# A first wave of 29 steps, and another order of a few loads and copies, in a spectral layer fused with a feed-forward layer

## The reference, cut to what matters

```
X = rfft(x, axis=1)
Yr = Xr @ w_r - Xi @ w_i + b_r ;  Yi = Xr @ w_i + Xi @ w_r + b_i
Y  = soft_threshold(Yr, 0.01) + 1j * soft_threshold(Yi, 0.01)
y  = irfft(Y, n=3008)
h  = y @ w_in
P  = a0 + a1*h + a2*h^2 + a3*h^3 ;  Q = 1 + |b0|*|h| + |b1|*h^2
out = (P / (Q + 1e-6)) @ w_out
```

## Time and profile before

| what | value |
|---|---|
| median of three runs | 1515.61 us |
| profiled execution: its time, its span | 1517.63 us, 1515.8 us |
| TensorE busy (matmuls) | 1452.0 us, 96% |
| VectorE busy | 1272.8 us, 84% |
| ScalarE busy | 1215.2 us, 80% |
| GpSimd busy | 636.8 us, 42% |
| moved by DMA | 187.90 MB, mean 124 GB/s |

### The profile page before, as it was taken

How to read it: one execution, slowest core, us unless ns; L and a number is a source line. 1 busy time by engine, 2 the same in 40 slices (tenths; PEclk the granted TensorE clock), 3 DMA queues, 4 the chain that set the end, 5 groups by cost and what they waited for, 6 DMA issues and landing times.

```text
span 1515.8 us, 19944 instructions
## 1 busy us (share of the span) xinstructions
PE 1452.0 (96%) x6976; PEld 1234.3 (81%) x6976; DVE 1272.8 (84%) x1301; ACT 1215.2 (80%) x1577; POOL 636.8 (42%) x420
## 2 busy tenths in 40 slices
PE   7996999999999999999999999999999999999986
PEld 2885888888888888888888888888888778787775
DVE  0243798888988888889899889989999999999997
ACT  3464788887888787888888888888888888888886
POOL 0000344444444444444444444444455555555554
PEclk9998999999999999999999999999999999999999
DMA  8875465665555655555554564555455544555443
GB/s 249 249 234 134 107 149 119 141 137 128 119 128 123 137 133 112 130 121 103 120 125 94 116 129 102 113 112 125 82 124 102 114 93 92 112 102 107 93 78 68
DMA packets 97682, 187.90 MB, mean 124 GB/s; under 512 B 11120, under 2 KB 57520, under 8 KB 97584
## 3 DMA queue, kind: packets, MB, share of 16 engines
q0 software_dynamic: 29952, 98.58, 35.4%
q1 hardware_dynamic: 67632, 88.05, 20.2%
HBM read 50.54 MB, written 37.49 MB: 58 GB/s over the span
## 4 chain that ended last, share of the span: by engine, by line
PE 65%; DVE 22%; issue 5%; DMA 4%; ACT 1%; SPq 1%; POOL 0%; POOLq 0%; ACTq 0%
PE h_ps L386 21%; PE o_ps L399 7%; PE o_ps L411 7%; PE o_ps L401 7%; DVE num L674 5%; DVE g_hi L666 5%; DVE den L669 5%; DVE num L649 5%; PE d L358 4%; PE d L359 4%; PE d L365 3%; PE d L371 3%; DMA zp_in<-spec 2%; PE d L345 2%; PE d L351 2%
## 5 line engine op out<-in xcount | busy, mean ns | idle before, releaser
L693 POOL TENSOR_TENSOR g_lo<-num,sq 128x940 fp32r<-128x940 f32 (+1 forms) x208 | 453.8, 2182 | 260.7 <-DVE num L674 260.4
L684 POOL DMA_DIRECT2D den<-sq x208 | 182.9, 879 | 612.5 <-PE o_ps L411 318.8
L399 PE MATMUL o_ps<-g_hi,wout_hi 128*128 128x470 f32 (+1 forms) x832 | 330.2, 398 | 0.0
L386 PE MATMUL h_ps<-yt_hi,win_hi 128*128 128x470 f32 (+1 forms) x832 | 312.1, 375 | 3.2 <-DVE num L654 3.2
L386 PE MATMUL h_ps<-yt_lo,win_hi 128*128 128x470 f32 (+1 forms) x832 | 311.5, 374 | 0.0
L386 PE MATMUL h_ps<-yt_hi,win_lo 128*128 128x470 f32 (+1 forms) x832 | 309.4, 372 | 0.0
L401 PE MATMUL o_ps<-g_hi,wout_lo 128*128 128x470 f32 (+1 forms) x832 | 309.1, 372 | 0.0
L411 PE MATMUL o_ps<-g_lo,wout_hi 128*128 128x470 f32 (+1 forms) x832 | 227.6, 395 | 30.1 <-POOL g_lo L693 30.0
L536 ACT ACTIVATE sq<-h_ps,bsq 128x940 f32<-128x940 f32 (+1 forms) x208 | 214.7, 1032 | 50.4 <-POOL g_lo L693 50.2
L666 DVE SCALAR_TENSOR_TENSOR g_hi<-num,a_sb,sq 128x940 fp32r<-128x940 f32 (+1 forms) x208 | 247.3, 1189 | 8.8 <-ACT sq L589 8.2
L674 DVE SCALAR_TENSOR_TENSOR num<-num,a_sb,den 128x940 f32<-128x940 f32 (+1 forms) x208 | 245.7, 1181 | 5.0
(11 more groups left out here) (64 smaller groups left out, 1498.7 us busy)
## 6 DMA issues: line engine op xcount, KB each, us to landing
den<-sq POOLq DMA_DIRECT2D x200, 470.0 KB, 4.4
spec<-s1w SPq DMA_DIRECT2D x64, 192.0 KB, 3.2
z_in<-spec SPq DMA_DIRECT2D x96, 128.0 KB, 3.3
spec<-s_out SPq DMA_DIRECT2D x96, 128.0 KB, 3.3
xw<-in_x SPq DMA_DIRECT2D x31, 384.0 KB, 4.4
out_t<-o_sb SPq DMA_DIRECT2D x25, 470.0 KB, 5.4
zp_in<-spec SPq DMA_DIRECT2D x22, 480.0 KB, 4.9
inv_in<-in_inv SPq DMA_DIRECT2D x96, 64.0 KB, 2.3
```

The source lines that it names most:

```text
L386: mm = pe.matmul(h_ps[q % 2][:, j, 0:cols(q)], w[:, h, f * P:(f + 1) * P], y[t % 2][:, h, 0:cols(q)], start=i == 0, stop=i == len(terms) - 1)
L399: pe.matmul(o_ps[:, h, 0:w], wout_hi[:, f, h * P:(h + 1) * P], g_hi[q % 2][:, j, 0:w], start=f == 0, stop=False)
L693: pool.tensor_tensor(g_lo[r % 2][:, :, 0:cols(r)], ring(num, r), ring(sq, r), ALU.mult).then_inc(n_g, 1)
```

## The change

PRE goes from 28 to 29: the wave has 29 spectral steps, and the slots have 67 (slot 38, the last of tile 4's four, is left empty). Three lists change beside it. SyncE loads w_r, w_i and the bias ahead of the first four z tiles instead of behind them. Of the four x chunks after the wave it issues one at once and three in slot 2, which puts them behind the z load of slot 1. On ScalarE group(1) is ahead of the loop beside group(0), and the copy of S2 of slot 0 is in slot 0, ahead of the reciprocal of slot 0, not at the head of slot 1.

```
-PRE = 28
+PRE = 29
...
-S2_SLOTS = (slots_at(range(5), (0, 2, 4, 6)) + slots_at(range(5, 10), (0, 2, 4, 6)) + slots_at([10], (0, 2, 4, 5))
+S2_SLOTS = (slots_at(range(4), (0, 2, 4, 6)) + slots_at([4], (0, 2, 4)) + slots_at(range(5, 10), (0, 2, 4, 6)) + slots_at([10], (0, 2, 4, 5))
...
             load_fwd(0)
-            for c in range(4):
-                load_z(c)
             load(wr_sb[:, :, :], w_r.rearrange("(h p) e -> p h e", p=P), s_wc)
             load(wi_sb[:, :, :], w_i.rearrange("(h p) e -> p h e", p=P), s_wc)
             load(bias_sb[:, :], bias, s_wc)
+            for c in range(4):
+                load_z(c)
...
             load_zp(1)
-            for k in range(S1N, S1N + 4):
-                load_x(k)
+            load_x(S1N)

             for q in range(NS + 3):
+                if q == 2:
+                    for k in range(S1N + 1, S1N + 4):
+                        load_x(k)
...
             group(0)
+            group(1)

             for q in range(NS + 2):
-                if q - 1 in S2_AT:
+                if q == 0 and q in S2_AT:
+                    evacuate_s2(S2_AT[q], d0[:, :])
+                if q - 1 in S2_AT and q >= 2:
                     evacuate_s2(S2_AT[q - 1], d0[:, :])
...
-                if q + 1 < NS:
+                if 1 <= q < NS - 1:
                     group(q + 1)
```

## The result

The changed kernel takes 1505.37 us (median of four runs, 1504.84 to 1506.35), the kernel before 1515.42 beside it; the ratio is 0.9933, 95% interval 0.9916 to 0.9950, so 10.2 us less by the ratio (7.6 to 12.7) and 10.05 by the medians. Forecast: 1505.4, range 1501.5 to 1510.5. A repetition gave 1505.06, ratio 0.9940 (0.9926 to 0.9953).

What follows compares the result with a forecast made beforehand. TensorE was taken to pace from 151 to 1090 us and VectorE after, so time won before 151 carries through. Terms 1.9 + 7.0 + 1.8 - 0.5 = 10.2 us gave a median of 1505.4, range 1501.5 to 1510.5.

Steps and rivals of the forecast that it cites:

- Term B: From zp_in at the wave's end through the first slots: 29th step, late chunks and earlier copy gain 7.0 us.
- term A: Start of the first wave: weights and bias loaded ahead of z gain 1.9 us (-0.5 to 3.5).
- its step from z to S3: Start of the wave: z issued at 29.2 takes 3.7, so S3 of step 0 starts 1.6 us sooner.
- The other part, the clock: Start of the wave: TensorE's half clock may end sooner or cover more work; 0.3 us (-0.7 to +1.0).
- Its first part: End of the wave: 29th step lies almost wholly inside the zp_in wait, so f1(0) starts 1.6 us sooner.
- now ScalarE's order decides: Slot 0: with the copy ahead of the reciprocal, S3 of slot 0 runs at 141.0, without waiting for den<-sq.
- Term C: Slot 38: dropped step saves TensorE 2.60 us, 0.75 goes back at slot 40; +1.8 (0.8 to 2.6).
- Term D: Slot 33: one more load issue ahead of zp_in lengthens TensorE's wait; -0.5 us (-1.0 to -0.2).
- The rule weighed: First slots: DMA engines take turns between queue rows, so fewer chunks ahead would not cure the late accumulate; given smaller chance.
- Rivals 1 and 2: First accumulate takes 11.1 us again, median 1508.1, chance 0.13; chunks delay the third, 3.4 lost, median 1508.8, chance 0.10.
- rival 5: Short gaps between 119 and 160 us keep TensorE at half clock: 4 us slower, median 1519.5, chance 0.02.
- rivals 3 and 4: Larger start or clock gains, 12 to 14 us, 1502.5, chance 0.14; VectorE or GpSimd paces, no measurable change, 1514, 0.06.

Runs made afterwards that it cites:

- e1: Kernel before with only w_r, w_i and the bias loaded ahead of the first four z tiles; 1516.32 us against 1516.23.
- e2: Kernel before with only PRE = 29 and the table of 67 steps; 1514.23 us, -2.1 us.
- e3: Kernel before with only ScalarE's copy of S2 of slot 0 moved ahead of the reciprocal; 1514.13 us, -2.3 us.
- e4: Kernel before with only the x chunks moved, one after the wave and three in slot 2; 1510.45 us, -5.9 us.
- again: The changed kernel unaltered, run again; 1505.06 us, -9.1 us against the kernel before.
- e5: Changed kernel with ScalarE's old order; 1505.82 us, -8.6 us against the kernel before.
- e6: Changed kernel with all four x chunks ahead of the slots; 1508.16 us, -6.2 us against the kernel before.
- e10: Changed kernel with slot 134 left out of the table instead of slot 38; 1506.82 us, -7.7 us against the kernel before.
- e11: Changed kernel with S2 of slot 0 in TensorE's wait for num and the three chunks in slot 3; 1505.19 us.
- e12: Changed kernel with S2 of slot 0 in TensorE's wait for num, chunks left in slot 2; 1508.57 us.
- e14: Changed kernel with two z loads first, then weights and bias, then two z loads; 1504.45 us.

## Why the prediction was right, point by point

**The time was right to 0.1 us, in part by luck: three of its four terms were off.** Term B was too small. What made up for it is only partly known, for term A can't be pinned down.

**Term A (+1.9): its step from z to S3 failed, and the term as a whole stays open.** The step that failed is "if z 0 is issued at 29.2 and takes 3.7": the z loads took 4.7, and 5.2 in e1. I had named this end ("z at 29.5 with 5.3 gives nothing") and taken the middle. From the z issue to S3 the new order takes 6.6 us (mean of eight profiles, 5.8 to 7.2), the old one 7.2 (mean of four): 0.6 us in place of 1.6. The loads do fill SyncE's wait, but the 640 KB then stand ahead of z, on engines that were 64 to 96% busy in each microsecond from 28 to 32 before as well.

The other part, the clock, had 0.3 in the forecast, and the profiles show more. Times in us, one number a profile:

| order of loads | z issue to S3 | S3 to zp_in's issue | together |
|---|---|---|---|
| old: before, e2, e3, e4 | 7.7, 6.8, 7.1, 7.2 | 80.6, 81.1, 80.8, 80.6 | 88.3, 87.9, 87.9, 87.8 |
| new: e1 | 7.2 | 79.6 | 86.8 |
| new: changed, again, e5, e6, e10, e11, e12 | 6.8, 7.2, 6.7, 6.5, 6.0, 6.7, 5.8 | 79.1, 79.3, 78.9, 78.7, 79.6, 78.6, 79.8 | 86.0, 86.5, 85.6, 85.1, 85.7, 85.3, 85.6 |

Behind S3 the new order takes 1.6 us less, and no profile of one order lies among those of the other. The granted clock is back at full 5.0 to 6.0 us after S3 in the old order and 1.2 to 3.5 us after it in the new one: in four of the eight (the changed kernel, its repetition, e1, e12) part of the half clock passes while TensorE waits for z, and in the other four it lasts 3.4 us, where it lasts 6.8 to 10.2 in the old order. In the mean 2.7 us less of half clock lie behind S3, and since at half clock a microsecond does half of its work, this accounts for 1.4 of the 1.6. With four profiles against eight I call that likely and not shown to follow from the order. So the profiles give A 2.1 us, nearly what I forecast, but by another way. The runs of e1 give it 0.3 (-1.5 to +1.1), and its profile, 1.1 ahead at zp_in's issue, is the smallest gain of the eight. What A is worth in the changed kernel lies between 0.3 and 2.1.

The two profiles shown differ by 3.4 us at the wave's end. 1.3 of them stood at the z issue, whose date is a draw in either order (26.4 to 28.8 us in the old one, 26.6 to 28.8 in the new); 0.9 arose up to S3 and 1.2 behind it, where the mean clock from 31.4 to 41.7 was 0.50 in the one and 0.73 in the other.

**Term B (+7.0) had the right mechanism and was too small.** Its first part, 1.6, was 2.4: S5 did not wait at all. In the profile of before alone it was 1.8 (10.8 us from zp_in's issue to f1(0)); the mean of its kind is 11.3, and I had read off one short draw of it. Its second part, 5.4, was 6.1 (39.1 to 33.0; 5.7 against the profile of before): the DMA, the copy and the reciprocal came as I worked them out, but TensorE waited 0.7 for g_lo, not 1.2. I had the copy 14.05 after f1(0) (140.3 less 126.25) and the end of g_lo 22.8 after it; measured 14.0 and 22.5.

**The shares within B were wrong.** I wrote "now ScalarE's order decides". It does not: e5, with the old order, can't be told from the changed kernel. With the chunks late, the copy and den<-sq come due within 2 us of each other, and it is all the same which goes first. The gain is the chunks' (e4, e6). I had credited two edits with one wait.

**Term C (+1.8) was 1.55** by the head start, with a wait of 0.4 for g_lo where I had placed 0.75. So 1.05 of the step's 2.60 went back, and 0.65 of that isn't traced to a wait. Whether the step would be worth as much elsewhere e10 leaves open.

**Term D (-0.5) was right**: the wait for zp_in at slot 34 is 0.75 where it was 0.43, and the head start falls by 0.34 (0.67 in the repetition), 0.5 in the mean. This is the row of the changed kernel:

```profile
380.83 1.32 PE L373 MATMUL d<-c_sb,zp_in 96*128 96x94 f32 x10 [0.75 <-DMA zp_in<-spec]
```

With A at 0.3, as e1's runs have it, the terms add up to 0.3 + 8.5 + 1.55 - 0.5 = 9.9; with the 2.1 of the profiles to 11.7. The measured 10.2 (7.6 to 12.7) and the repetition's 9.1 (7.1 to 11.2) are nearer the first.

**The rule weighed.** By the trace of before I took the accumulate to stand behind the chunks. e12 has it the other way round, the chunks behind the accumulate, with nearly the same delay and both queues at 72 and 40% in the same microsecond, 38 and 39 packets. There this trace agrees with the rule of the Trainium skill, "DMA: Bandwidth & Descriptors" (queues, rings and completion order), that an engine takes turns between queue rows. From 135 to 136 us there are 87 packets of the hardware queue to 9 of the other, though the first accumulate lands only at 138.1 and the second, issued at 131.0, after 10.1 us: even turns are not what that microsecond shows. But my conclusion from it, that fewer chunks would then not help, was wrong: who has to share is slower too, and e4 gains 5.9 us. What the rule does not tell is that the software queue of the kernel before moved nothing from 134 to 139 us: its first data came 5 us after the issue, and 4.7 us after it in e6, in the changed kernel 2.8 us after it. In e12 it was 3.0: chunks issued behind the accumulate don't put off its start, they slow it once it runs. Chunks ahead of it do put off its start. Why it starts late beside a full hardware queue is open.

**Rivals 1 and 2** did not come: the first den<-sq landed after 6.3, the third after 4.7 us. Nor did the half clock of rival 5: the mean clock from 119 to 160 us was 0.96. The times of rivals 3 and 4 (1502.5 and 1514) lie outside the four runs.

## What to carry to other kernels

When two edits end the same wait, the sum over the edits is not the gain. Ask of each what it is worth when the other is done, and leave one out at a time. A load that is moved into idle time of the *issuing* engine brings its user little sooner if the queues behind it are full (0.6 us here); count the bytes ahead of the last thing needed, and put only those ahead (e14, whose first use came sooner, though its runs show no gain). A dead wait at the end of a phase that has a fixed date, here the landing of zp_in, is the place for a step of the next phase (e2). And one profile of each kernel is one draw: that term A has a second part came out only when twelve were laid side by side.

## What the runs showed of the hardware

An accumulating DMA of 470 KB on the software queue lands after 4.4 us in the steady state, 5.9 to 7.3 behind zp_in and one chunk of 384 KB, and 9.9 to 11.1 with three chunks more, even where all three are issued half a microsecond behind it. A z load of 128 KB took 2.4 to 2.6 us (the median of the first four) in the four profiles with nothing new ahead of it, and 3.5 to 5.5 in the eight with 640 KB issued ahead. Near the first z loads TensorE's granted clock stood at half for 3.4 us in some profiles and for up to 10.2 in others. I had not expected the spread of the runs either: 29 runs of the kernel before on one chip lie between 1513.5 and 1520.3 us, the nine of the changed kernel, from two other series, between 1504.6 and 1506.4. How much of that arises at the start no trace here splits off.
